# Two matmul pairs of the down products change places: the g_lo products of the main accumulators go behind the g_hi products of the rest accumulators

## The chip, the cores and the metric

The kernel runs on one core of a Trainium2 chip. The core has a matrix engine (TensorE, PE in the profile, with its weight loads shown apart as PEld), VectorE (DVE), ScalarE (ACT), GpSimd (POOL), and SyncE (SP), which here issues the DMAs. Each engine works through its own queue in order, and the queues meet at semaphores. The metric is the device time of one launch in microseconds; less is better.

## What is computed

Three stages over 8192 tokens of width 192. First a causal convolution over 7 tokens with one softmax weight per head and tap, then two feed-forward layers of width 2048 with different activations, in fp32:

```python
out = np.einsum('hk,bskhg->bshg', w, x_unf)          # 7 taps, 8 heads
h = x @ w_in                                         # layer 1: 192 -> 2048
g = np.where(pos, h, np.where(neg, 0.0, (h + beta) ** 2 / (4.0 * beta)))
x = g @ w_out                                        # 2048 -> 192
h = x @ w_in2                                        # layer 2
g = h * (1.0 / (1.0 + np.exp(-1.702 * h)))
return (g @ w_out2).astype(np.float32)
```

## The kernel before

The tokens are cut into 16 tiles of 512. Everything lies transposed: features on the partitions, tokens along the free axis. A feed-forward layer takes 16 steps per tile, one for every 128 of its 2048 hidden features. A step has an up product (into one of the PSUM banks `h`), the activation, and a down product that adds into two banks which last for the whole tile: `main` for output features 0 to 127 and `rest` for the remaining 64.

To keep fp32 precision with the faster fp32r matmuls, operands are split in a rounded part (hi) and a residue (lo). ScalarE rounds the activated tile to g_hi, VectorE subtracts to get g_lo. A down step is then main += w_main g_hi + w_lo g_hi + w_main g_lo, and rest += w_rest g_hi + w_rest g_lo (`w_rest` holds hi and lo weights side by side in 128 columns).

Layer 2 runs `BEHIND` = 24 steps behind layer 1. After the first 24 steps both layers are at work in every slot, and TensorE pairs them. It does not use its 128 rows for one product: the contraction over 128 partitions is cut into LOWER (partitions 0 to 63) and UPPER (64 to 127), and each matmul uses 64 rows. While LOWER works on layer 1, UPPER works on layer 2, and in the second half of a product they change over. In the code the two matmuls of such a pair stand one behind the other (`main1`, `main2`, ...). Since one layer's two halves add into the same bank, the second half of a bank may begin only when the other rows' last matmul on that bank is done. This is what the semaphores `main_half`, `main2_half`, `rest_half` and `rest2_half` are for.

In a slot TensorE does `end_up` (10 matmuls: second half of the up products), `begin_up` (8: first half of the next ones) and `down_both` (20: both halves of the down products, for steps two slots back, `LAG`). `down_both` is lines 616 to 676. The first half of the down products is L634 to L660: L634, L647, L650, L655 and L659 are LOWER (layer 1), L646, L648, L652, L658 and L660 are UPPER (layer 2). The second half is L664 to L676, where layer 1 is UPPER (L664, L667, L669, L672, L675) and layer 2 LOWER (L666, L668, L670, L674, L676). The order within each queue is written out by hand; no scheduler has a part in it.

Who feeds the down step: ScalarE's `round_gate1` (L796) writes g_hi of layer 1, VectorE's `residue1` (L976) writes g_lo of layer 1 and raises `g1_lo_ready`, `residue2` (L982) g_lo of layer 2 and `g2_lo_ready`. At the first step of a tile the bank `main1` must have been read by VectorE (L992) and `rest1` too (L996, y_part), both counted by `y_from_dve`; for layer 2 `out_copied` and `out_summed` do this. GpSimd computes the convolution for the tile after next alongside, in bursts.

`down_both` runs 231 times: 6 slots ahead of the loop, 192 in the loop (6 passes of two tiles with 16 slots each), and 33 behind it.

Of the kernel before, what the change touches and what calls it, by code (L numbers as in the profile page):

```python
# [19 lines left out]
def conv_mlp_mlp(nc, x, conv_w, w_in1, w_out1, w_in2, w_out2, out):  # L20
# [42 lines left out]
    with ExitStack() as ctx:  # L63
# [3 lines left out]
        def sem(name):  # L67
            return ctx.enter_context(nc.semaphore(name))
# [70 lines left out]
        g1_lo_ready = sem("g1_lo_ready")  # L139
# [5 lines left out]
        main_half = sem("main_half")  # L145
        rest_half = sem("rest_half")
        main2_half = sem("main2_half")
# [3 lines left out]
        g2_lo_ready = sem("g2_lo_ready")  # L151
# [60 lines left out]
        LOWER, UPPER = slice(0, DR), slice(DR, P)  # L212
# [94 lines left out]
        def chunk_of(m, kind, c):  # L307
            return m * N_CHUNKS + CHUNKS.index((kind, c))
# [202 lines left out]
        def _(pe):  # L511
# [104 lines left out]
            def down_both(one, two):  # L616

                first1, last1 = one.s == 0, one.s == F_TILES - 1
                first2, last2 = two.s == 0, two.s == F_TILES - 1
                w1, w2 = w_down[0][:, one.s, :], w_down[1][:, two.s, :]  # L620
                hi1, lo1 = g1_hi[one.s % G_RING], g1_lo[one.s % G_RING]
                hi2, lo2 = g2_hi[two.s % G_RING], g2_lo[two.s % G_RING]
                w1_main, w1_rest, w1_lo = w1[:, 0:DM], w1[:, DM:DM + 2 * DR], w1[:, D + DR:2 * D]
                w2_main, w2_rest, w2_lo = w2[:, 0:DM], w2[:, DM:DM + 2 * DR], w2[:, D + DR:2 * D]
                main1, rest1 = (t[:, :] for t in acc1)
                main2, rest2 = (t[:, :] for t in acc2)
                later2 = not isinstance(two.n, int) or two.tile > 0

                pe.wait_ge(g1_hi_ready, one.n + 1)

                pe.wait_ge(down1_done, one.n)
                if first1:
                    pe.wait_ge(y_from_dve, one.tile * 3 - 2)
                nc.tensor.matmul(main1, w1_main[LOWER, :], hi1[LOWER, :], start=first1, stop=False)  # L634
                if isinstance(two.n, int) and two.tile == 0 and two.s % OUT_CHUNK == 0:
                    pe.wait_ge(wp_ready, chunk_of(1, "out", two.s // OUT_CHUNK) + 1 - DVE_CHUNKS)
                pe.wait_ge(g2_hi_ready, two.n + 1)
                if later2 or two.s > 0:

                    pe.wait_ge(down2_done, two.n)  # L640
                else:

                    pe.wait_ge(x_from_dve, 4)
                if first2 and later2:
                    pe.wait_ge(out_copied, two.tile * 2 - 1)
                nc.tensor.matmul(main2, w2_main[UPPER, :], hi2[UPPER, :], start=first2, stop=False)  # L646
                nc.tensor.matmul(main1, w1_lo[LOWER, :], hi1[LOWER, :], start=False, stop=False)  # L647
                nc.tensor.matmul(main2, w2_lo[UPPER, :], hi2[UPPER, :], start=False, stop=False)  # L648
                pe.wait_ge(g1_lo_ready, one.n + 1)
                nc.tensor.matmul(main1, w1_main[LOWER, :], lo1[LOWER, :], start=False, stop=False).then_inc(main_half, 1)  # L650
                pe.wait_ge(g2_lo_ready, two.n + 1)
                nc.tensor.matmul(main2, w2_main[UPPER, :], lo2[UPPER, :], start=False, stop=False).then_inc(main2_half, 1)  # L652
                if first1:
                    pe.wait_ge(y_from_dve, one.tile * 3 - 1)
                nc.tensor.matmul(rest1, w1_rest[LOWER, :], hi1[LOWER, :], start=first1, stop=False)  # L655
                if first2 and later2:
                    pe.wait_ge(out_summed, two.tile)
                nc.tensor.matmul(rest2, w2_rest[UPPER, :], hi2[UPPER, :], start=first2, stop=False)  # L658
                nc.tensor.matmul(rest1, w1_rest[LOWER, :], lo1[LOWER, :], start=False, stop=False).then_inc(rest_half, 1)  # L659
                nc.tensor.matmul(rest2, w2_rest[UPPER, :], lo2[UPPER, :], start=False, stop=False).then_inc(rest2_half, 1)  # L660


                pe.wait_ge(main_half, one.n - (BEHIND - 1))
                nc.tensor.matmul(main1, w1_main[UPPER, :], hi1[UPPER, :], start=False, stop=False)  # L664
                pe.wait_ge(main2_half, two.n + 1)
                nc.tensor.matmul(main2, w2_main[LOWER, :], hi2[LOWER, :], start=False, stop=False)  # L666
                nc.tensor.matmul(main1, w1_lo[UPPER, :], hi1[UPPER, :], start=False, stop=False)  # L667
                nc.tensor.matmul(main2, w2_lo[LOWER, :], hi2[LOWER, :], start=False, stop=False)  # L668
                nc.tensor.matmul(main1, w1_main[UPPER, :], lo1[UPPER, :], start=False, stop=last1)  # L669
                nc.tensor.matmul(main2, w2_main[LOWER, :], lo2[LOWER, :], start=False, stop=last2)  # L670
                pe.wait_ge(rest_half, one.n - (BEHIND - 1))
                nc.tensor.matmul(rest1, w1_rest[UPPER, :], hi1[UPPER, :], start=False, stop=False)  # L672
                pe.wait_ge(rest2_half, two.n + 1)
                nc.tensor.matmul(rest2, w2_rest[LOWER, :], hi2[LOWER, :], start=False, stop=False)  # L674
                nc.tensor.matmul(rest1, w1_rest[UPPER, :], lo1[UPPER, :], start=False, stop=last1).then_inc(down1_done, 1)  # L675
                nc.tensor.matmul(rest2, w2_rest[LOWER, :], lo2[LOWER, :], start=False, stop=last2).then_inc(down2_done, 1)  # L676

# [65 lines left out]
            def slot(tile, side, s):  # L743
                if is_solo(tile, s):
                    solo_slot(tile, side, s)
                    return
                n = tile * F_TILES + s if isinstance(tile, int) else None
                if n is not None and n >= ALL_STEPS:
                    tail_slot(tile, side, s)
                    return  # L750
                if n is None or n > BEHIND:
                    end_up(back(tile, side, s, 1), back(tile, side, s, BEHIND + 1))
                begin_up(back(tile, side, s, 0), back(tile, side, s, BEHIND))
                if n is None or n >= BEHIND + LAG:
                    down_both(back(tile, side, s, LAG), back(tile, side, s, BEHIND + LAG))

            def tail_slot(tile, side, s):
                n = tile * F_TILES + s
                two = back(tile, side, s, BEHIND)
                if n == ALL_STEPS:  # L760
                    end_up(back(tile, side, s, 1), back(tile, side, s, BEHIND + 1))
                    down_both(back(tile, side, s, LAG), back(tile, side, s, BEHIND + LAG))
                if two is not None:
                    up2(two)
                if n == ALL_STEPS + 1:
                    down1(back(tile, side, s, LAG))
                if n > ALL_STEPS:
                    down2(back(tile, side, s, BEHIND + LAG))
# [404 lines left out]
```

## Time and profile before

| | us |
|---|---|
| median of 3 runs | 1221.22 (1221.20 to 1223.06) |
| profiled execution, whole | 1221.22 |
| profiled execution, span | 1219.4 |
| PE busy | 1178.3 (97%) |
| PEld busy | 1067.6 (88%) |
| DVE busy | 889.0 (73%) |
| ACT busy | 819.7 (67%) |
| POOL busy | 471.4 (39%) |

The mean granted TensorE clock was 0.988 of full speed, with the lower values in the first slices. The table's shares are averages over the whole span. A matmul row gives the start and a modelled end; matmuls overlap in the array (each of 0.39 us, one begun every 0.23 us in each half of the rows), so what tells the pace is the distance between starts in one half, not the busy time. A weight load (PEld) has the line of the matmul that it belongs to.

### The profile page before, as it was taken

The numbers are of one execution on the slowest core, as the hardware profiler recorded it, in microseconds if no ns is written. First come the engines' busy times: TensorE is split into PE (matmuls) and PEld (weight loads), VectorE is DVE, ScalarE is ACT, GpSimd is POOL, SyncE is SP. The second block draws the span as 40 slices with busy tenths as digits, with TensorE's granted clock in tenths as the row PEclk, the third lists the DMA queues.
The fourth block names the chain that finished last, engine by engine and source line by source line (L and its number), as shares of the span: only waits on it lengthen the run. The fifth ranks groups of instructions, "written<-read, shape, count | busy, mean of one in ns | idle before, by whom it ended". The sixth has DMA issues, their size and how long they took to land.

```text
span 1219.4 us, 25844 instructions
## 1 busy us (share of the span) xinstructions
PE 1178.3 (97%) x9326; PEld 1067.6 (88%) x9326; DVE 889.0 (73%) x1205; ACT 819.7 (67%) x1545; POOL 471.4 (39%) x426
## 2 busy tenths in 40 slices
PE   7998899999999999999999999999999999999995
PEld 3776798999989899898989989899998989999974
DVE  6976768687786877869687786868778696766532
ACT  5866676776757677685766758576675767765542
POOL 5859818054170714508072360906327080000000
PEclk8999899999999999999999999999999999999998
DMA  7221010101010010101001010000101000000001
GB/s 173 74 67 59 1 34 12 36 1 47 1 46 1 9 39 1 47 1 23 25 7 41 1 47 1 14 33 4 44 1 46 2 11 5 3 13 1 14 10 17
DMA packets 63569, 30.87 MB, mean 25 GB/s; under 512 B 56052, under 2 KB 60274, under 8 KB 63472
## 3 DMA queue, kind: packets, MB, share of 16 engines
q1 hardware_dynamic: 63472, 29.40, 9.5%
q8 instruction: 82, 1.34, 0.4%
q14 instruction: 15, 0.12, 0.0%
HBM read 23.09 MB, written 6.29 MB: 24 GB/s over the span
## 4 chain that ended last, share of the span: by engine, by line
PE 70%; DVE 10%; ACT 7%; issue 6%; POOL 5%; DMA 1%; DVEq 0%; SPq 0%; ACTq 0%; POOLq 0%
ACT clip L790 3%; DVE g_lo L976 3%; DVE g_lo L982 3%; PE acc L650 3%; PE acc L634 2%; PE acc L676 2%; PE acc L655 2%; PE acc L659 2%; PE acc L668 2%; PE acc L674 2%; PE acc L670 2%; PE acc L666 2%; DVE clip L961 2%; PE h L604 2%; PE h L576 2%
## 5 line engine op out<-in xcount | busy, mean ns | idle before, releaser
L790 ACT ACTIVATE clip<-clip,half 128x512 f32<-128x512 f32 x256 | 186.1, 727 | 126.1 <-DVE clip L961 116.8
L970 DVE TENSOR_TENSOR gate<-h,clip 128x512 f32<-128x512 f32 x232 | 160.5, 692 | 143.5 <-ACT clip L790 139.4
L804 ACT ACTIVATE g_hi<-h 128x512 fp32r<-128x512 f32 x256 | 153.5, 600 | 141.9 <-PE h L613 114.5
L982 DVE TENSOR_TENSOR g_lo<-gate,g_hi 128x512 fp32r<-128x512 f32 x256 | 214.9, 839 | 34.0 <-ACT gate L808 34.0
L976 DVE TENSOR_TENSOR g_lo<-gate,g_hi 128x512 fp32r<-128x512 f32 x232 | 223.5, 963 | 18.6 <-ACT g_hi L796 4.4
L961 DVE TENSOR_SCALAR clip<-h 128x512 f32<-128x512 f32 x256 | 175.2, 684 | 84.4 <-PE h L611 79.3
L423 POOL TENSOR_TENSOR x_conv<-x_in,tap_w 128x384 f32<-128x384 f32 (+2 forms) x30 | 26.3, 897 | 499.7 <-ACT raw L844 496.6
L430 POOL TENSOR_TENSOR x_conv<-x_conv,prod 128x384 f32<-128x384 f32 (+2 forms) x180 | 215.9, 1218 | 1.6
L796 ACT ACTIVATE g_hi<-gate 128x512 fp32r<-128x512 f32 x232 | 147.1, 634 | 79.0 <-DVE gate L970 74.4
L423 POOL TENSOR_TENSOR prod<-x_in,tap_w 128x384 f32<-128x384 f32 (+2 forms) x180 | 193.6, 1096 | 8.0 <-DMA x_in<-in_x 3.3
L808 ACT ACTIVATE gate<-h 128x512 f32<-128x512 f32 x256 | 148.7, 581 | 0.0
L844 ACT ACTIVATE raw<-x_conv 32x128 f32<-32x128 f32 x336 | 103.8, 309 | 6.2 <-POOL x_conv L430 1.6
L650 PE MATMUL acc<-g_lo,w_down 64*128 64x512 f32 x231 | 95.8, 415 | 4.4 <-DVE g_lo L976 4.3
L652 PE MATMUL acc<-g_lo,w_down 64*128 64x512 f32 x231 | 95.2, 412 | 0.0
L634 PE MATMUL acc<-g_hi,w_down 64*128 64x512 f32 x231 | 92.2, 399 | 1.7 <-ACT g_hi L796 1.6
L646 PE MATMUL acc<-g_hi,w_down 64*128 64x512 f32 x231 | 91.8, 397 | 0.0
L664 PE MATMUL acc<-g_hi,w_down 64*128 64x512 f32 x231 | 90.8, 393 | 0.0
L659 PE MATMUL acc<-g_lo,w_down 64*128 64x512 f32 x231 | 90.8, 393 | 0.0
L668 PE MATMUL acc<-g_hi,w_down 64*128 64x512 f32 x231 | 90.6, 392 | 0.0
L667 PE MATMUL acc<-g_hi,w_down 64*128 64x512 f32 x231 | 90.6, 392 | 0.0
L655 PE MATMUL acc<-g_hi,w_down 64*128 64x512 f32 x231 | 90.6, 392 | 0.0
L660 PE MATMUL acc<-g_lo,w_down 64*128 64x512 f32 x231 | 90.6, 392 | 0.0
(253 smaller groups left out, 4798.1 us busy)
## 6 DMA issues: line engine op xcount, KB each, us to landing
x_in<-in_x SPq DMA_DIRECT2D x14, 960.0 KB, 4.7
out_y<-raw SPq DMA_DIRECT2D x384, 16.0 KB, 1.4
raw<-in_moe_w_out SPq DMA_DIRECT2D x6, 384.0 KB, 3.3
raw<-in_moe_w_in SPq DMA_DIRECT2D x4, 512.0 KB, 7.5
raw<-in_moe_w_in SPq DMA_DIRECT2D x8, 256.0 KB, 7.2
stage<-in_moe_w_out SPq DMA_DIRECT2D x2, 384.0 KB, 15.1
x_in<-in_x SPq DMA_DIRECT2D x1, 768.0 KB, 4.7
x_in<-in_x SPq DMA_DIRECT2D x2, 283.5 KB
```

What stands on the lines that cost most here:

```text
L423: ins = nc.gpsimd.tensor_tensor(by_head(dst, j), by_head(x_in, at + j), w, ALU.mult)
L430: ins = nc.gpsimd.tensor_tensor(o, o, prod[k % 2][:, j:j + slabs, 0:width], ALU.add)
L634: nc.tensor.matmul(main1, w1_main[LOWER, :], hi1[LOWER, :], start=first1, stop=False)
L650: nc.tensor.matmul(main1, w1_main[LOWER, :], lo1[LOWER, :], start=False, stop=False).then_inc(main_half, 1)
L790: nc.scalar.activation(c, c, ACT.Square, bias=half[:, :], scale=0.5).then_inc(square_ready, 1)
L796: nc.scalar.activation(g1_hi[step.s % G_RING][:, :], gate1_of(step)[:, :], ACT.Copy).then_inc(g1_hi_ready, 1)
L804: nc.scalar.activation(g2_hi[step.s % G_RING][:, :], src, ACT.Gelu_apprx_sigmoid).then_inc(g2_hi_ready, 1)
L808: nc.scalar.activation(gate2[:, :], src, ACT.Gelu_apprx_sigmoid).then_inc(gate2_ready, 1)
L961: nc.vector.tensor_scalar(clip[step.s % 2][:, :], bank1(step)[:, :], -1.0, 1.0, ALU.max, ALU.min).then_inc(clip_ready, 1)
L970: nc.vector.tensor_tensor(gate1_of(step)[:, :], bank1(step)[:, :], clip[step.s % 2][:, :], ALU.max).then_inc(gate1_ready, 1)
L976: nc.vector.tensor_tensor(g1_lo[k][:, :], gate1_of(step)[:, :], g1_hi[k][:, :].bitcast(FP32), ALU.subtract).then_inc(g1_lo_ready, 1)
L982: nc.vector.tensor_tensor(g2_lo[k][:, :], gate2[:, :], g2_hi[k][:, :].bitcast(FP32), ALU.subtract).then_inc(g2_lo_ready, 1)
```

## The change

In `down_both`, in the first half, the pair of g_lo products into the main banks (with the waits for `g1_lo_ready` and `g2_lo_ready`, and with the increments of `main_half` and `main2_half`) moves behind the pair of g_hi products into the rest banks (with their waits at a tile's first step). In the second half the same pairs change places, there without waits of their own on g_lo; the waits for `rest_half` and `rest2_half` move ahead with the rest pair. No instruction is added or removed.

```diff
--- before.py
+++ after.py
@@ -646,16 +646,16 @@
                 nc.tensor.matmul(main2, w2_main[UPPER, :], hi2[UPPER, :], start=first2, stop=False)
                 nc.tensor.matmul(main1, w1_lo[LOWER, :], hi1[LOWER, :], start=False, stop=False)
                 nc.tensor.matmul(main2, w2_lo[UPPER, :], hi2[UPPER, :], start=False, stop=False)
-                pe.wait_ge(g1_lo_ready, one.n + 1)
-                nc.tensor.matmul(main1, w1_main[LOWER, :], lo1[LOWER, :], start=False, stop=False).then_inc(main_half, 1)
-                pe.wait_ge(g2_lo_ready, two.n + 1)
-                nc.tensor.matmul(main2, w2_main[UPPER, :], lo2[UPPER, :], start=False, stop=False).then_inc(main2_half, 1)
                 if first1:
                     pe.wait_ge(y_from_dve, one.tile * 3 - 1)
                 nc.tensor.matmul(rest1, w1_rest[LOWER, :], hi1[LOWER, :], start=first1, stop=False)
                 if first2 and later2:
                     pe.wait_ge(out_summed, two.tile)
                 nc.tensor.matmul(rest2, w2_rest[UPPER, :], hi2[UPPER, :], start=first2, stop=False)
+                pe.wait_ge(g1_lo_ready, one.n + 1)
+                nc.tensor.matmul(main1, w1_main[LOWER, :], lo1[LOWER, :], start=False, stop=False).then_inc(main_half, 1)
+                pe.wait_ge(g2_lo_ready, two.n + 1)
+                nc.tensor.matmul(main2, w2_main[UPPER, :], lo2[UPPER, :], start=False, stop=False).then_inc(main2_half, 1)
                 nc.tensor.matmul(rest1, w1_rest[LOWER, :], lo1[LOWER, :], start=False, stop=False).then_inc(rest_half, 1)
                 nc.tensor.matmul(rest2, w2_rest[UPPER, :], lo2[UPPER, :], start=False, stop=False).then_inc(rest2_half, 1)
 
@@ -666,12 +666,12 @@
                 nc.tensor.matmul(main2, w2_main[LOWER, :], hi2[LOWER, :], start=False, stop=False)
                 nc.tensor.matmul(main1, w1_lo[UPPER, :], hi1[UPPER, :], start=False, stop=False)
                 nc.tensor.matmul(main2, w2_lo[LOWER, :], hi2[LOWER, :], start=False, stop=False)
-                nc.tensor.matmul(main1, w1_main[UPPER, :], lo1[UPPER, :], start=False, stop=last1)
-                nc.tensor.matmul(main2, w2_main[LOWER, :], lo2[LOWER, :], start=False, stop=last2)
                 pe.wait_ge(rest_half, one.n - (BEHIND - 1))
                 nc.tensor.matmul(rest1, w1_rest[UPPER, :], hi1[UPPER, :], start=False, stop=False)
                 pe.wait_ge(rest2_half, two.n + 1)
                 nc.tensor.matmul(rest2, w2_rest[LOWER, :], hi2[LOWER, :], start=False, stop=False)
+                nc.tensor.matmul(main1, w1_main[UPPER, :], lo1[UPPER, :], start=False, stop=last1)
+                nc.tensor.matmul(main2, w2_main[LOWER, :], lo2[LOWER, :], start=False, stop=last2)
                 nc.tensor.matmul(rest1, w1_rest[UPPER, :], lo1[UPPER, :], start=False, stop=last1).then_inc(down1_done, 1)
                 nc.tensor.matmul(rest2, w2_rest[LOWER, :], lo2[LOWER, :], start=False, stop=last2).then_inc(down2_done, 1)
```

First place, TensorE's queue in the first half of `down_both` in a loop slot, from the third pair on. acc1_0 is main1, acc1_1 rest1, acc2_0 main2, acc2_1 rest2. Before:

```order
L650 MATMUL acc1_0<-g1_lo1,w_down1 128x512 [waits g1_lo_ready]
L652 MATMUL acc2_0<-g2_lo1,w_down2 128x512 [waits g2_lo_ready]
L655 MATMUL acc1_1<-g1_hi1,w_down1 128x512
L658 MATMUL acc2_1<-g2_hi1,w_down2 128x512
L659 MATMUL acc1_1<-g1_lo1,w_down1 128x512
L660 MATMUL acc2_1<-g2_lo1,w_down2 128x512
```

and now (the lines are those of the changed file):

```order
L651 MATMUL acc1_1<-g1_hi1,w_down1 128x512
L654 MATMUL acc2_1<-g2_hi1,w_down2 128x512
L656 MATMUL acc1_0<-g1_lo1,w_down1 128x512 [waits g1_lo_ready]
L658 MATMUL acc2_0<-g2_lo1,w_down2 128x512 [waits g2_lo_ready]
L659 MATMUL acc1_1<-g1_lo1,w_down1 128x512
L660 MATMUL acc2_1<-g2_lo1,w_down2 128x512
```

The pair that waits for g_lo stood third and stands fourth; the next pair to wait, for `main_half` and `main2_half`, stood three pairs behind it and now stands two pairs behind it.

Second place, the same queue right behind, the second half of `down_both`. Before:

```order
L664 MATMUL acc1_0<-g1_hi1,w_down1 128x512 [waits main_half]
L666 MATMUL acc2_0<-g2_hi1,w_down2 128x512 [waits main2_half]
L667 MATMUL acc1_0<-g1_hi1,w_down1 128x512
L668 MATMUL acc2_0<-g2_hi1,w_down2 128x512
L669 MATMUL acc1_0<-g1_lo1,w_down1 128x512
L670 MATMUL acc2_0<-g2_lo1,w_down2 128x512
L672 MATMUL acc1_1<-g1_hi1,w_down1 128x512 [waits rest_half]
L674 MATMUL acc2_1<-g2_hi1,w_down2 128x512 [waits rest2_half]
L675 MATMUL acc1_1<-g1_lo1,w_down1 128x512
L676 MATMUL acc2_1<-g2_lo1,w_down2 128x512
```

and now:

```order
L664 MATMUL acc1_0<-g1_hi1,w_down1 128x512 [waits main_half]
L666 MATMUL acc2_0<-g2_hi1,w_down2 128x512 [waits main2_half]
L667 MATMUL acc1_0<-g1_hi1,w_down1 128x512
L668 MATMUL acc2_0<-g2_hi1,w_down2 128x512
L670 MATMUL acc1_1<-g1_hi1,w_down1 128x512 [waits rest_half]
L672 MATMUL acc2_1<-g2_hi1,w_down2 128x512 [waits rest2_half]
L673 MATMUL acc1_0<-g1_lo1,w_down1 128x512
L674 MATMUL acc2_0<-g2_lo1,w_down2 128x512
L675 MATMUL acc1_1<-g1_lo1,w_down1 128x512
L676 MATMUL acc2_1<-g2_lo1,w_down2 128x512
```

The rest pair with its two waits stood fourth of five and stands third; the last pair, whose end frees the operands and the banks, is where it was.

## Rows read from the trace of the kernel before

**Rows 1.** The page: busy us, share of the span, instructions of each engine.
```profile
PE 1178.3 (97%) x9326; PEld 1067.6 (88%) x9326; DVE 889.0 (73%) x1205; ACT 819.7 (67%) x1545; POOL 471.4 (39%) x426
```

**Rows 2.** The page, costliest groups: the g_lo matmul of LOWER.
```profile
L650 PE MATMUL acc<-g_lo,w_down 64*128 64x512 f32 x231 | 95.8, 415 | 4.4 <-DVE g_lo L976 4.3
```

**Rows 3.** Timeline of a quiet slot: start us, duration us, engine, line, operation.
```profile
600.86 0.39 PE L634 MATMUL acc<-g_hi,w_down 64*128 64x512 f32 x1
...
601.10 0.39 PE L647 MATMUL acc<-g_hi,w_down 64*128 64x512 f32 x1
...
601.41 0.39 PE L652 MATMUL acc<-g_lo,w_down 64*128 64x512 f32 x1
...
601.79 0.39 PE L659 MATMUL acc<-g_lo,w_down 64*128 64x512 f32 x1
601.86 0.18 PEld L666 LDWEIGHTS acc<-g_hi,w_down 64*128 64x128 f32 x1
601.88 0.39 PE L660 MATMUL acc<-g_lo,w_down 64*128 64x512 f32 x1
...
602.03 0.39 PE L666 MATMUL acc<-g_hi,w_down 64*128 64x512 f32 x1
...
602.11 0.39 PE L664 MATMUL acc<-g_hi,w_down 64*128 64x512 f32 x1
...
605.30 0.39 PE L634 MATMUL acc<-g_hi,w_down 64*128 64x512 f32 x1
```

**Rows 4.** List of waits, of weight loads: us in total, times, longest.
```profile
PEld acc L650 <- DVE g_lo L976: 21.9, 64, 0.9
```

**Rows 5.** Timeline of the slot with the longest wait of a tile.
```profile
560.18 0.39 PE L647 MATMUL acc<-g_hi,w_down 64*128 64x512 f32 x1
...
560.88 0.18 PEld L650 LDWEIGHTS acc<-g_lo,w_down 64*128 64x128 f32 x1 [0.74 <-DVE g_lo L976]
560.88 0.50 PE L650 MATMUL acc<-g_lo,w_down 64*128 64x512 f32 x1 [0.31 <-DVE g_lo L976]
560.89 0.18 PEld L652 LDWEIGHTS acc<-g_lo,w_down 64*128 64x128 f32 x1
...
561.23 0.39 PE L655 MATMUL acc<-g_hi,w_down 64*128 64x512 f32 x1
```

**Rows 6.** Timeline of the slot after it.
```profile
565.19 0.39 PE L647 MATMUL acc<-g_hi,w_down 64*128 64x512 f32 x1
...
565.38 0.18 PEld L650 LDWEIGHTS acc<-g_lo,w_down 64*128 64x128 f32 x1 [0.23 <-DVE g_lo L976]
...
565.72 0.39 PE L655 MATMUL acc<-g_hi,w_down 64*128 64x512 f32 x1
```

**Rows 7.** Timeline of PE: start and end of the waiting slots.
```profile
555.42 0.39 PE L634 MATMUL acc<-g_hi,w_down 64*128 64x512 f32 x1
...
578.21 0.39 PE L590 MATMUL h<-x_rest_a,rest_hi 64*128 64x512 f32 x1
```

**Rows 8.** Timeline of VectorE, its g_lo of the first layer.
```profile
539.98 0.69 DVE L976 TENSOR_TENSOR g_lo<-gate,g_hi 128x512 fp32r<-128x512 f32 x1
...
545.12 0.69 DVE L976 TENSOR_TENSOR g_lo<-gate,g_hi 128x512 fp32r<-128x512 f32 x1
...
559.33 1.50 DVE L976 TENSOR_TENSOR g_lo<-gate,g_hi 128x512 fp32r<-128x512 f32 x1
...
563.83 1.50 DVE L976 TENSOR_TENSOR g_lo<-gate,g_hi 128x512 fp32r<-128x512 f32 x1
...
572.82 1.50 DVE L976 TENSOR_TENSOR g_lo<-gate,g_hi 128x512 fp32r<-128x512 f32 x1
```

**Rows 9.** Timeline of the slot that begins a token tile in rest1.
```profile
578.47 0.67 DVE L996 TENSOR_TENSOR y_part<-acc,y_part 64x512 f32<-64x512 f32 x1
...
578.94 0.39 PE L647 MATMUL acc<-g_hi,w_down 64*128 64x512 f32 x1
...
579.19 0.18 PEld L655 LDWEIGHTS acc<-g_hi,w_down 64*128 64x128 f32 x1
```

## The prediction

> **What bounds the kernel now.** I read the page first for the engine that fills the span. TensorE is busy 1178.3 us of 1219.4 [rows 1], VectorE 73%, so any time lost or won on TensorE's queue counts at once, while the others have room. Next I read the timeline of one quiet slot (one pass of the PE queue: end of an up product, start of the next, and the 20 down matmuls) [rows 3]. From one L634 to the next are 605.30 - 600.86 = 4.44 us. That is 38 matmuls, 19 in each half of the array (LOWER rows 0 to 63, UPPER rows 64 to 127), and the halves run side by side: 4.44 / 19 = 0.234 us from one matmul to the next in the same half. The reader should see in these rows that L634 (600.86) and L647 (601.10) are both LOWER and 0.24 apart, that the UPPER half follows 0.08 us later (L659 at 601.79, L660 at 601.88), and that nothing idles. So a quiet slot is at its floor, and only two things can move the time: a stall that goes and a stall that comes.
>
> The stalls that are there I took from the list of waits: the weight load of L650 waits for VectorE's g_lo in 64 slots, 21.9 us in all [rows 4]. It is one of 231 such slots [rows 2]. The wait stands at the weight load, not at the matmul; that matters below. I then looked at the worst such slot [rows 5] and a mild one [rows 6] to learn what a late load costs:
> - Worst: L647 starts at 560.18, the load of L650 only at 560.88, and L655, two places on, at 561.23 instead of 560.18 + 0.47 = 560.65. So a load is followed by the next matmul of its half but one 0.35 us later; with the usual 0.234 taken off, a matmul really streams about 0.115 us after its load begins.
> - Mild: load 0.19 late (565.38 after 565.19), L655 at 565.72, which is 0.53 after L647 instead of 0.47: 0.06 lost. The same rule gives 0.19 + 0.115 - 0.234 = 0.07.
> The rule I take: a load may start up to 0.12 us after the matmul before it in its half at no cost; every ns beyond that is lost.
> A second thing in rows 5: L652 is UPPER and waits for another semaphore, yet its load starts at 560.89, 0.01 after L650's. Waits are taken in program order, and one held load holds those behind it in both halves.
>
> How much these stalls are worth in a tile of 16 slots: from L634 at 555.42 to L590 at 578.21 [rows 7] lie five slots less one matmul, 94 intervals of 0.234 = 21.9 to 22.0 us; they took 22.79. About 0.8 us per tile is lost, over 64 / 5 = 13 tiles (five waiting slots each): 10.4 us, the most that moving L650 can give back.
>
> **What the change removes.** The g_lo matmul moves behind the hi matmul of the rest accumulator, in each half one interval later, so it tolerates 0.23 us more lateness of VectorE. The lower bound of the gain is this one shift per tile, since the lateness of a tile is one run of slots: 13 x 0.23 = 3.0 us. The upper bound is all of it, 10.4 us. Which one depends on who sets the pace in these slots. VectorE does [rows 8]: its g_lo (L976) takes 0.69 us early and 1.50 us later. It ends at 540.67 (539.98 + 0.69) and, four slots on, at 560.83 (559.33 + 1.50): 5.04 us per slot, 0.6 more than TensorE's 4.44, so VectorE falls behind. After that it runs at (572.82 - 563.83) / 2 = 4.50. If TensorE's own slot grows to 4.54 (next part), 4 x 0.1 = 0.4 us less lateness comes together in the four slots, and VectorE's 4.50 is then the faster of the two. With the 0.23 of the shift that is 0.63, against the 0.58 lost in the worst slot (1.05 - 0.47) [rows 5]. So I take all of it: -10.4 us.
>
> **What the change adds.** The second half of the down products may touch an accumulator's bank only when the first half's last matmul on it is done: L664 (UPPER) waits for main_half, L666 (LOWER) for main2_half. In the quiet slot [rows 3] L652 starts at 601.41, ends at 601.80, and the load of L666 starts at 601.86: 0.45 after L652, and 0.07 after L659, its neighbour in LOWER. It is waiting already, inside the free 0.12. After the change L650 and L652 start one interval (0.234) later and L664, L666 stay where they are. Step by step, with T the start of L634 in its half: the g_lo matmul starts at T + 3 x 0.234 = T + 0.70; the load that waits for it at T + 1.15; the matmul streams from T + 1.265; its place was T + 5 x 0.234 = T + 1.17. Lost: 0.10 us. With the present lead of 0.08 of LOWER over UPPER the first such slot costs LOWER 0.17 and UPPER 0.02, which brings the halves level or over; since a held load holds both, they settle level, at 0.10 each in every slot. Bounds per slot: 0 (if a late load cost nothing) and 0.17 (if the lagging half set the pace every time). I take 0.10, by the nearest rows, those of 5 and 6: 231 x 0.10 = +23.1 us.
>
> The Trainium skill, page "TensorE: Matmul & The Clock Gate", section "Architectural detail: the array is 16× 32×32, not 1× 128×128", says that a matmul can begin before its weight load has finished. By that alone the late load would be free. The record agrees as to the start (L650 is recorded at 560.88 with its load [rows 5]) but it lasts 0.50 instead of 0.39 and the next matmul comes 0.35 after the load, so the measurement decides for a cost.
>
> The waits of the rest accumulators: rest_half comes at the same matmul as before (L659), its waiter moves one interval ahead. L659 at T + 0.93, plus 0.45 = T + 1.38; the load's place is T + 1.40 without, T + 1.50 with the new stall. It costs 0 while the stall before it covers it.
>
> Once a tile, rest1's first matmul waits for y_part (L996) and is now one interval earlier. L996 ends at 578.47 + 0.67 = 579.14 [rows 9], and L655's load starts at 579.19. In the new place it would be due at L647's start, 578.94: 0.25 late, less the free 0.12 = 0.13; 13 to 14 tiles, x 0.12 = +1.6 us. Bounds 0 and 14 x 0.23 = 3.2. The wait of rest2 for out_summed is due earlier by as much, and no such wait is in the list, so 0. Loads, matmuls, DMAs and the work of the other engines stay the same in number. The last pair of the second half keeps its place, so down1_done and down2_done, on which ScalarE waits, do not move within a slot.
>
> Sum: +23.1 - 10.4 + 1.6 = +14.3 us. The profiled execution took 1221.22 (1219.4 span and 1.8 around it), the same as the median, so 1221.2 + 14.3 = 1235.5. In the first few down slots TensorE waits for others anyway, which may hide up to 7 x 0.10 = 0.7.
>
> **The rivals.**
> - A, faster: the late load of the second half costs nothing. For it: the load would be 0.21 late, still inside the 0.234 interval. It decides if the load may be hidden up to 0.23 instead of 0.12. Then +23.1 and the y_part cost go, VectorE keeps its pace of 4.50 in five slots, and only the shift is won: 1221.2 - 3.0 = 1218.2. Against it: rows 6, where 0.19 late cost 0.06. The sentence of the Trainium skill cited above would lead here. Chance 0.06.
> - B, much slower: the halves do not settle level; the one that lags pays 0.17 in every slot and the other waits for it. 231 x 0.17 = 39.3, - 10.4 + 1.6 = +30.5: 1251.7. Against it: the halves have separate streams in rows 3. Chance 0.06.
> - C, about the same: the completion signal is nearer than 0.45 because the last matmul on a bank drains while others run, and the stall is 0.04: 231 x 0.04 = 9.2, - 8 + 1 = +2: 1223.4. Here TensorE stays faster than 4.50, so less than 10.4 is won back. Chance 0.06.
> - D: the stall is as forecast but VectorE still is late and only 3.0 is won: 1221.2 + 23.1 - 3.0 + 1.6 = 1242.9. For it: the 0.63 of slack against 0.6 needed is thin. Chance 0.12, with all between it and the forecast.
>
> **How the numbers follow.** Forecast 0.70, its own range 1230 to 1240 (0.08 to 0.12 per slot). The range reaches to D: 1228 to 1243; A, B and most of C are left out. 0.2% is 2.4 us, about what a measurement of this kernel can tell from no change. Faster: A, 0.05. Same: the weak end of A and half of C, 0.04. Slower: the rest, 0.91.
>
> **What would show it.** A quiet slot, L634 to L634, at 4.53 to 4.54 us instead of 4.44. The loads of L664 and L666 0.21 after the matmul before them in their half (0.45 after the moved g_lo matmuls), the halves nearly level. The list of waits with little or nothing for g_lo at the moved matmul, and new waits at L664 and L666 for matmuls of TensorE itself. VectorE's total busy time as before. The forecast is wrong if a quiet slot still takes 4.44 us (then A), or over 4.6 (then B); if it takes 4.53 and g_lo is still waited for, it is D.

## The result, and the profile after

| | before | changed |
|---|---|---|
| median, us | 1221.68 (4 runs) | 1236.43 (4 runs) |
| ratio | | 1.0116, 95% interval 1.0099 to 1.0134 |
| span of the profiled execution | 1219.4 | 1235.4 |

The change costs 14.8 us. 1235.5 was forecast, with a range of 1228 to 1243.

The page of the changed kernel: first the busy times (answers to [rows 1]), then the costliest groups (line, engine, operation, tiles, count | busy us, mean ns | idle before, releaser).

```profile
PE 1198.1 (97%) x9326; PEld 1040.4 (84%) x9326; DVE 890.0 (72%) x1205; ACT 817.4 (66%) x1545; POOL 471.3 (38%) x426
...
L666 PE MATMUL acc<-g_hi,w_down 64*128 64x512 f32 x231 | 115.3, 499 | 0.0
L664 PE MATMUL acc<-g_hi,w_down 64*128 64x512 f32 x231 | 113.7, 492 | 0.0
...
L664 PEld LDWEIGHTS acc<-g_hi,w_down 64*128 64x128 f32 x231 | 42.4, 184 | 59.7 <-PE acc L656 59.6
```

TensorE's matmuls are "busy" 20 us longer, but not because there is more to do: the count is the same. L666 and L664 have a mean of 499 and 492 ns where a matmul that nothing holds has 391, because the record of a matmul whose load came late begins with the load. The third of these group rows tells why the loads come late: 59.7 us of idle weight-load time before L664, ended by L656, which is a matmul of TensorE itself.

The list of waits of the weight loads (us in total, times, longest), against [rows 4]:

```profile
PEld acc L664 <- PE acc L656: 59.6, 230, 0.3
...
PEld acc L651 <- DVE y_part L996: 2.5, 11, 0.2
...
PEld acc L656 <- DVE g_lo L976: 1.8, 5, 0.6
...
PEld acc L634 <- DVE y_lo_a L992: 1.2, 6, 0.2
...
PEld acc L634 <- DVE y_lo_b L992: 1.0, 5, 0.2
```

The wait for g_lo was 21.9 us in 64 slots and is 1.8 in 5 (it stands at L656 now). In its place is a wait of TensorE for its own other half, 59.6 us in 230 of 231 slots. Before, a tile's first slot waited at L634 for y_lo longer than now, and not at all for y_part:

```profile
PEld acc L634 <- DVE y_lo_b L992: 2.7, 6, 0.5
PEld acc L634 <- DVE y_lo_a L992: 2.6, 6, 0.4
```

How late g_lo comes is seen best in the slot with the longest wait of a tile. First the kernel before, where the g_lo of rows 8 ends at 559.33 + 1.50 = 560.83, then the same slot of the changed kernel:

```profile
559.95 0.39 PE L634 MATMUL acc<-g_hi,w_down 64*128 64x512 f32 x1
```

```profile
565.95 1.50 DVE L976 TENSOR_TENSOR g_lo<-gate,g_hi 128x512 fp32r<-128x512 f32 x1
567.07 0.39 PE L634 MATMUL acc<-g_hi,w_down 64*128 64x512 f32 x1
```

Before, g_lo is ready 0.88 us after the slot's L634; now 565.95 + 1.50 - 567.07 = 0.38 after it. That is 0.50 less, and the load that needs it is due 0.47 after L634 now instead of 0.23.

A quiet slot of the changed kernel (start us, duration us, engine, line, operation), against [rows 3]:

```profile
621.81 0.39 PE L646 MATMUL acc<-g_hi,w_down 64*128 64x512 f32 x1
...
621.85 0.39 PE L634 MATMUL acc<-g_hi,w_down 64*128 64x512 f32 x1
...
622.55 0.39 PE L656 MATMUL acc<-g_lo,w_down 64*128 64x512 f32 x1
...
622.75 0.39 PE L660 MATMUL acc<-g_lo,w_down 64*128 64x512 f32 x1
...
623.00 0.18 PEld L664 LDWEIGHTS acc<-g_hi,w_down 64*128 64x128 f32 x1 [0.26 <-PE acc L656]
623.00 0.49 PE L664 MATMUL acc<-g_hi,w_down 64*128 64x512 f32 x1
623.03 0.18 PEld L666 LDWEIGHTS acc<-g_hi,w_down 64*128 64x128 f32 x1
623.03 0.50 PE L666 MATMUL acc<-g_hi,w_down 64*128 64x512 f32 x1
...
623.34 0.39 PE L667 MATMUL acc<-g_hi,w_down 64*128 64x512 f32 x1
...
623.37 0.39 PE L668 MATMUL acc<-g_hi,w_down 64*128 64x512 f32 x1
...
626.40 0.39 PE L634 MATMUL acc<-g_hi,w_down 64*128 64x512 f32 x1
```

The g_lo matmul on main of layer 1's first half, L656, starts at 622.55, and the load that waits for it at 623.00: 0.45 later, as the held load in [rows 3]. The load stands 0.25 after the matmul before it in its half (L660, 622.75), and the next matmul of the half, L667, comes 0.34 after the load. From L660 to L667 are 0.59 instead of 0.47: 0.12 lost. UPPER is 0.03 to 0.04 us ahead of LOWER through the slot, and the two held loads start 0.03 apart. From L634 (621.85) to L634 (626.40) are 4.55 us.

**All slots.** Over the 230 intervals between the 231 slots, from the rows of L634 (min/median/max duration, then first and last start us), before and changed:

```profile
L634 PE MATMUL acc<-g_hi,w_down x231: 390/391/625, 97.2 to 1143.0; 64*128 64x512 f32 x116
```

```profile
L634 PE MATMUL acc<-g_hi,w_down x231: 390/392/789, 98.1 to 1159.0; 64*128 64x512 f32 x116
```

1143.0 - 97.2 = 1045.8 us before, 1159.0 - 98.1 = 1060.9 now: 15.1 of the 16.0 us of span lie here. The mean slot is 4.547 and 4.613; the median of the same intervals, which leaves out the stalls of once a tile, is 4.434 and 4.553.

### The profile page after: what moved, and what is told of

The parts are those of the page before. It is cut to its first block, busy times and chain, and to the rows that moved or that the text cites. A ratio compares the mean times of both kernels' runs of the same rounds, so it can differ in the third digit from the quotient of the medians.

```text
span 1235.4 us, 25844 instructions
## 1 busy us (share of the span) xinstructions
PE 1198.1 (97%) x9326; PEld 1040.4 (84%) x9326; DVE 890.0 (72%) x1205; ACT 817.4 (66%) x1545; POOL 471.3 (38%) x426
## 4 chain that ended last, share of the span: by engine, by line
PE 89%; POOL 5%; ACT 2%; DVE 2%; DMA 1%; issue 1%; SPq 0%; POOLq 0%; ACTq 0%; DVEq 0%
PE acc L664 6%; PE acc L673 4%; PE h L587 4%; PE h L607 4%; PE acc L675 4%; PE h L605 4%; PE h L589 4%; PE h L609 4%; PE h L585 4%; PE acc L670 4%; PE h L611 4%; PE h L602 4%; PE h L592 4%; PE acc L648 4%; PE acc L667 3%; PE acc L646 3%
## 5 line engine op out<-in xcount | busy, mean ns | idle before, releaser
L976 DVE TENSOR_TENSOR g_lo<-gate,g_hi 128x512 fp32r<-128x512 f32 x232 | 223.7, 964 | 19.3 <-ACT g_hi L796 5.2
L666 PE MATMUL acc<-g_hi,w_down 64*128 64x512 f32 x231 | 115.3, 499 | 0.0
L664 PE MATMUL acc<-g_hi,w_down 64*128 64x512 f32 x231 | 113.7, 492 | 0.0
L634 PE MATMUL acc<-g_hi,w_down 64*128 64x512 f32 x231 | 91.5, 396 | 2.5 <-ACT g_hi L796 2.5
L664 PEld LDWEIGHTS acc<-g_hi,w_down 64*128 64x128 f32 x231 | 42.4, 184 | 59.7 <-PE acc L656 59.6
L651 PE MATMUL acc<-g_hi,w_down 64*128 64x512 f32 x231 | 92.4, 400 | 0.0
L646 PE MATMUL acc<-g_hi,w_down 64*128 64x512 f32 x231 | 91.8, 398 | 0.0
L658 PE MATMUL acc<-g_lo,w_down 64*128 64x512 f32 x231 | 91.5, 396 | 0.0
L656 PE MATMUL acc<-g_lo,w_down 64*128 64x512 f32 x231 | 91.0, 394 | 0.3 <-DVE g_lo L976 0.2
L654 PE MATMUL acc<-g_hi,w_down 64*128 64x512 f32 x231 | 91.2, 395 | 0.0
L648 PE MATMUL acc<-g_hi,w_down 64*128 64x512 f32 x231 | 91.2, 395 | 0.0
```

Source lines behind the costliest of these rows:

```text
L976: nc.vector.tensor_tensor(g1_lo[k][:, :], gate1_of(step)[:, :], g1_hi[k][:, :].bitcast(FP32), ALU.subtract).then_inc(g1_lo_ready, 1)
```

## The experiments

The first four ran on one chip together. "One wait instead of two" (both_waits below), "The new order in the waiting slots alone" (late_slots_only) and "VectorE's lateness taken away at its source" (x_early) shared a second chip, "The pair swapped" and "The change and the earlier x together" a third. A ratio compares with the kernel before on the same chip. The diffs are shortened: `...` stands for what is left out, and so do comments; waits that go along with a matmul are not all printed.

### First half alone

```diff
-                nc.tensor.matmul(main1, ..., lo1[LOWER, :], ...).then_inc(main_half, 1)
-                nc.tensor.matmul(main2, ..., lo2[UPPER, :], ...).then_inc(main2_half, 1)
                 nc.tensor.matmul(rest1, ..., hi1[LOWER, :], ...)
                 nc.tensor.matmul(rest2, ..., hi2[UPPER, :], ...)
+                nc.tensor.matmul(main1, ..., lo1[LOWER, :], ...).then_inc(main_half, 1)
+                nc.tensor.matmul(main2, ..., lo2[UPPER, :], ...).then_inc(main2_half, 1)
```

> Only the first half of the down products is reordered (g_lo pair of main behind the g_hi pair of rest), the second half as before. Theory (the bank handover at L664 and L666 is what costs): all of the cost is here, a quiet slot of 4.55 us as in the changed kernel, g_lo no longer waited for, about 1236 us (1234 to 1238). Rival (the alternation between banks in each half costs some 0.06 us per half): 4.49 us per slot and about 1229.

Measured: 1235.5 us, ratio 1.0118 (1.0101 to 1.0134). The waits of its weight loads:

```profile
PEld acc L664 <- PE acc L656: 59.3, 230, 0.3
```

All of the cost is in the first half's order: the wait is the changed kernel's (59.6), and the median slot is 4.547 us. The rival falls.

### Second half alone

```diff
-                nc.tensor.matmul(main1, ..., lo1[UPPER, :], ..., stop=last1)
-                nc.tensor.matmul(main2, ..., lo2[LOWER, :], ..., stop=last2)
                 nc.tensor.matmul(rest1, ..., hi1[UPPER, :], ...)
                 nc.tensor.matmul(rest2, ..., hi2[LOWER, :], ...)
+                nc.tensor.matmul(main1, ..., lo1[UPPER, :], ..., stop=last1)
+                nc.tensor.matmul(main2, ..., lo2[LOWER, :], ..., stop=last2)
```

> Only the second half is reordered, the first as before. Theory: rest_half and rest2_half are signalled 0.45 us after L659 and L660, at T+1.38 and T+1.46, and the loads that wait are due at T+1.40, inside the free 0.12 us: nothing lost, slot 4.43, g_lo waited for as before (about 22 us in 64 slots), 1221 to 1223 us. Rival (alternation costs in each half): about 1229.

Measured: 1221.6 us, ratio 1.0001 (0.9992 to 1.0011). The wait for g_lo is as it was:

```profile
PEld acc L650 <- DVE g_lo L976: 22.2, 65, 0.8
```

The second half's order and the rest accumulators' earlier waits cost nothing: the median slot stays 4.434 us.

### One place further

```diff
 # first half, against the kernel before; the g_hi pair of rest now follows directly here
-                pe.wait_ge(g1_lo_ready, one.n + 1)
-                nc.tensor.matmul(main1, ..., lo1[LOWER, :], ...).then_inc(main_half, 1)
-                pe.wait_ge(g2_lo_ready, two.n + 1)
-                nc.tensor.matmul(main2, ..., lo2[UPPER, :], ...).then_inc(main2_half, 1)
 ...
+                pe.wait_ge(g1_lo_ready, one.n + 1)
                 nc.tensor.matmul(rest1, ..., lo1[LOWER, :], ...).then_inc(rest_half, 1)
+                pe.wait_ge(g2_lo_ready, two.n + 1)
                 nc.tensor.matmul(rest2, ..., lo2[UPPER, :], ...).then_inc(rest2_half, 1)
+                nc.tensor.matmul(main1, ..., lo1[LOWER, :], ...).then_inc(main_half, 1)
+                nc.tensor.matmul(main2, ..., lo2[UPPER, :], ...).then_inc(main2_half, 1)
```

> First half: the g_lo pair of main goes one more place back, behind the g_lo pair of rest, so that the bank is handed over with one pair between instead of two; second half as before. Theory (signal 0.45 us after the last matmul on the bank, then 0.12 us free): one interval of 0.234 us more per slot than in the changed kernel, 4.79 us per slot, 1236 + 54 = 1290 us (1285 to 1295). Rival (a fixed cost of any wait that is met late, whatever the distance): 1236.

Counted from the pair that signals to the pair that waits, the distance is three pairs in the kernel before, two in the changed kernel and one here. So two pairs, one and none stand between them; the expectation above, and the one of the next experiment, count one too many where they say "between".

Measured: 1283.19 us (one run). In a quiet slot (L659 is the last matmul on main of LOWER here):

```profile
618.55 0.39 PE L634 MATMUL acc<-g_hi,w_down 64*128 64x512 f32 x1
...
619.49 0.39 PE L659 MATMUL acc<-g_lo,w_down 64*128 64x512 f32 x1
619.93 0.18 PEld L664 LDWEIGHTS acc<-g_hi,w_down 64*128 64x128 f32 x1 [0.48 <-PE acc L659]
...
623.33 0.39 PE L634 MATMUL acc<-g_hi,w_down 64*128 64x512 f32 x1
```

The load of L664 starts 0.44 after L659, and the slot takes 4.78 us: 0.23 more than the changed kernel's (4.55). By the medians it is 4.773 against 4.553. Taking one pair out of the distance costs about one interval, and the signal keeps its way of 0.44 to 0.45. The time came 7 us lower than forecast: 231 x 0.22 is 51 instead of 54, and the rest fits the once-a-tile stalls that are left in the changed kernel: the wait for y_part, 2.5 us in 11 slots there, is 0.2 in one here.

### Distance restored

```diff
 # down_both, between its two halves, on top of the change; end_up later leaves this pair out
+                pe.wait_ge(h1_half, one.n - (BEHIND - 1))
+                nc.tensor.matmul(bank_1, in_hi[0][UPPER, cols1], x_hi[UPPER, :], start=False, stop=False)
+                pe.wait_ge(h2_half, two.n + 1)
+                nc.tensor.matmul(bank_2, in_hi[1][LOWER, cols2], y_hi[LOWER, :], start=False, stop=False)
```

> The changed kernel, with the first pair of the next up product's second half (L602, L604) moved between the two halves of the down products, so that main is handed over with three pairs between, as before. Nothing added or removed. Theory: the stall at L664 goes, quiet slot 4.43; g_lo keeps its 0.23 us of tolerance (-3.0), the last down pair ends 0.23 us later, which the handover of a tile's banks to VectorE waits for (+3.0, once a tile), y_part +1.5: 1220 to 1225 us. Rival (the order of the products as such costs): 4.55 per slot and 1236 or more.

Measured: 1224.64 us, ratio 1.003 (1.002 to 1.0039). In a quiet slot (L659 is the g_lo matmul into main of LOWER, L669 the first UPPER matmul of the second half):

```profile
623.88 0.39 PE L659 MATMUL acc<-g_lo,w_down 64*128 64x512 f32 x1
...
624.37 0.18 PEld L669 LDWEIGHTS acc<-g_hi,w_down 64*128 64x128 f32 x1
...
624.60 0.39 PE L669 MATMUL acc<-g_hi,w_down 64*128 64x512 f32 x1
```

L669's load is 0.49 after L659 and the matmul follows 0.23 after its load: not late. The median slot is 4.441 us. 11 of the 15 us are gone although the down products stand in the changed order, so the distance is what costs. The time is at the upper end of what was expected. The wait for g_lo did not shrink:

```profile
PEld acc L659 <- DVE g_lo L983: 22.2, 66, 0.7
```

against 21.9 in 64 before, so the 3.0 us that the forecast gave to the shift did not come. The last down pair ends one interval later here, ScalarE's copy of the output comes after it, and VectorE waits for that copy (L1005; L1012 in this file): 17.8 us in 15 times against 14.5 in 15 before, 0.22 more each time. In the slot with the longest wait g_lo ends 1.10 us after the slot's first down matmul (L983 at 559.37 + 1.50, L637 at 559.77) instead of 0.88. VectorE is later by what the shift gives, and the two cancel. A tile's first load waits longer for y_lo too, 7.3 us in all instead of 5.3.

### One wait instead of two

```diff
                 pe.wait_ge(main_half, one.n - (BEHIND - 1))
-                nc.tensor.matmul(main1, w1_main[UPPER, :], hi1[UPPER, :], start=False, stop=False)
                 pe.wait_ge(main2_half, two.n + 1)
+                nc.tensor.matmul(main1, w1_main[UPPER, :], hi1[UPPER, :], start=False, stop=False)
```

> The changed kernel, but the waits for main_half and main2_half both stand ahead of L664, and L666 has none of its own. The changed kernel's slot is 4.553 us, 0.12 over 4.434, where 0.10 was forecast; its halves stand 0.035 us apart with UPPER ahead, and the held loads of L664 and L666 start 0.034 apart. Theory 1 (two held loads one behind the other are let go 0.034 apart, and the half that is let go last is the one that L664 waits for in the next slot): with one held load the halves come level and the slot shrinks by 0.02 to 0.035, to 4.52 to 4.535, 1229 to 1233 us. Theory 2 (the signal is simply later than 0.45 us): slot 4.55 and 1236 as in the changed kernel.

Measured: 1257.18 us, ratio 1.0293 (1.0271 to 1.0315), 21 us slower than the changed kernel; both theories miss it.

```profile
622.78 0.39 PE L658 MATMUL acc<-g_lo,w_down 64*128 64x512 f32 x1
...
622.82 0.39 PE L656 MATMUL acc<-g_lo,w_down 64*128 64x512 f32 x1
...
623.36 0.18 PEld L665 LDWEIGHTS acc<-g_hi,w_down 64*128 64x128 f32 x1 [0.35 <-PE acc L656]
...
623.39 0.18 PEld L666 LDWEIGHTS acc<-g_hi,w_down 64*128 64x128 f32 x1
...
623.70 0.39 PE L667 MATMUL acc<-g_hi,w_down 64*128 64x512 f32 x1
```

The held load starts 0.54 after L656 instead of 0.45, so two waits ahead of one load cost 0.09 to 0.10 us per slot, x 231 = 21 to 23; the median slot is 4.653. The second signal is not what comes late: L658, which gives it, starts 0.04 before L656. The halves still stand 0.04 apart and the loads 0.03, though only one of them has waits: theory 1 falls. Theory 2 left the number of waits out of account, so this run does not test it.

### The pair swapped

```diff
-                pe.wait_ge(main_half, one.n - (BEHIND - 1))
-                nc.tensor.matmul(main1, w1_main[UPPER, :], hi1[UPPER, :], start=False, stop=False)
                 pe.wait_ge(main2_half, two.n + 1)
                 nc.tensor.matmul(main2, w2_main[LOWER, :], hi2[LOWER, :], start=False, stop=False)
+                pe.wait_ge(main_half, one.n - (BEHIND - 1))
+                nc.tensor.matmul(main1, w1_main[UPPER, :], hi1[UPPER, :], start=False, stop=False)
```

> The changed kernel with L666 (LOWER, layer 2) ahead of L664 (UPPER, layer 1) in the queue, each with its own wait. Theory (of two held loads the second starts 0.034 later whatever it waits for, and in the next slot the first one waits for the half that lags): mirror image, LOWER now 0.035 ahead, slot again 4.55, 1236 us. Rival (the 0.02 over the forecast belongs to UPPER or to main_half's signal): slot 4.53, about 1231.

Measured: 1236.83 us (one run). L664 is the LOWER and L666 the UPPER matmul here, L656 LOWER, L658 UPPER:

```profile
621.85 0.39 PE L656 MATMUL acc<-g_lo,w_down 64*128 64x512 f32 x1
...
621.86 0.39 PE L658 MATMUL acc<-g_lo,w_down 64*128 64x512 f32 x1
...
622.33 0.18 PEld L664 LDWEIGHTS acc<-g_hi,w_down 64*128 64x128 f32 x1 [0.29 <-PE acc L658]
...
622.34 0.18 PEld L666 LDWEIGHTS acc<-g_hi,w_down 64*128 64x128 f32 x1
```

The time is the one forecast, but the picture is not the mirror image: the halves stand level (0.01), and the loads start 0.47 and 0.49 after the matmuls that they wait for. The median slot is the changed kernel's, 4.553. The same 0.03 us is paid, once as a distance between the halves and once as a later signal. What it is stays open.

### The new order in the waiting slots alone

```diff
+                late = one.s in (11, 12, 13, 14, 15)
+                if late:   # with the waits of this pair at a tile's first step
+                    nc.tensor.matmul(rest1, ..., hi1[LOWER, :], ...)
+                    nc.tensor.matmul(rest2, ..., hi2[UPPER, :], ...)
                 nc.tensor.matmul(main1, ..., lo1[LOWER, :], ...).then_inc(main_half, 1)
                 nc.tensor.matmul(main2, ..., lo2[UPPER, :], ...).then_inc(main2_half, 1)
-                nc.tensor.matmul(rest1, ..., hi1[LOWER, :], ...)
-                nc.tensor.matmul(rest2, ..., hi2[UPPER, :], ...)
+                if not late:
+                    nc.tensor.matmul(rest1, ..., hi1[LOWER, :], ...)
+                    nc.tensor.matmul(rest2, ..., hi2[UPPER, :], ...)
```

> Before, with the first half's new order only in the five slots of a tile in which VectorE's g_lo is waited for (layer 1 steps 11 to 15, TensorE slots 13, 14, 15, 0 and 1). Theory: in the worst slot 0.23 of the 0.51 us of stall goes, the five slots pay the 0.12 of the bank handover, but there TensorE stands waiting for VectorE anyway; quiet slots stay at 4.43. Net -0.3 to +0.1 us per tile, 1217 to 1223 us. Rival (the cost of the new order comes on top everywhere): five times 0.12 more per tile, 13 tiles, less 3.0: 1226 or more.

Measured: 1222.76 us, ratio 1.0016 (1.0006 to 1.0027). In its file L660 is the g_lo matmul and L675 the first of the second half:

```profile
PEld acc L675 <- PE acc L660: 18.0, 73, 0.3
PEld acc L660 <- DVE g_lo L987: 8.3, 19, 0.8
```

The wait for g_lo fell from 21.9 to 8.3 us, and 18.0 us of waits for the bank came in 73 slots. The time lies inside the range of the theory, at its upper end, and the median slot is 4.437 us. The new order takes away much of the wait that it was put there for and gives the time back next to it; nothing is won even where it works.

### VectorE's lateness taken away at its source

```diff
-        EARLY = dict(move=..., turn={7: 0, 10: 1}, hi={10: 0, 11: 1},
-                     lo={11: 0, 12: 1})
+        EARLY = dict(move=..., turn={7: 0, 10: 1}, hi={8: 0, 11: 1},
+                     lo={9: 0, 12: 1})
```

> The kernel before, TensorE's order untouched; of the preparation of the next tile's x the rounding of the main part on ScalarE moves from slot 10 to 8 and its residue on VectorE (L1028, 0.75 us) from slot 11 to 9, ahead of the stretch in which GpSimd works and VectorE's g_lo takes 1.5 us. Theory (the wait at L650 is accumulated lateness of VectorE, 0.6 us by slot 14): the lateness shrinks by the 0.7 us that leave the stretch, the wait in slots 13 and 14 goes and most of that in 15 to 1 with it: 0.5 to 0.8 us per tile, 1211 to 1215 us. Rival (VectorE's lateness is set in slot 9 by its wait for the output copy, L1005, and an operation more there makes it worse): 1221 or more.

Measured: 1215.26 us, ratio 0.9958 (0.9945 to 0.9971), faster than both kernels. VectorE (against [rows 8]) and the wait at L650:

```profile
539.18 0.67 DVE L1028 TENSOR_TENSOR x_lo_a<-raw,x_hi_a 128x512 fp32r<-128x512 f32 x1
...
541.50 0.69 DVE L976 TENSOR_TENSOR g_lo<-gate,g_hi 128x512 fp32r<-128x512 f32 x1
...
555.25 1.50 DVE L976 TENSOR_TENSOR g_lo<-gate,g_hi 128x512 fp32r<-128x512 f32 x1
```

```profile
PEld acc L650 <- DVE g_lo L976: 15.0, 54, 0.8
```

L1028 stands in slot 9 now. From the end of the L976 at 541.50 (542.19) to the end of the one at 555.25 (556.75) are three slots of 4.85 us. In the kernel before, the three that end at 560.83 begin at 545.81 [rows 8] and average 5.01. VectorE takes 0.46 us less for three slots. In the worst slot its g_lo ends 0.53 us after L634 (556.75 and 556.22) instead of 0.88, the slot ahead of that one no longer waits, and the wait fell from 21.9 to 15.0 us. The time is 0.3 us above the range that was expected (1211 to 1215); the slots after the worst wait as before, since VectorE runs at 4.50 there.

### The change and the earlier x together

```diff
 # on top of the change
-                     turn={7: 0, 10: 1}, hi={10: 0, 11: 1}, lo={11: 0, 12: 1}
+                     turn={7: 0, 10: 1}, hi={8: 0, 11: 1}, lo={9: 0, 12: 1}
```

> The changed kernel with x_early's edit. Theory (in the changed kernel VectorE is late nowhere any more, all of that gain is taken, and the slot of 4.55 is TensorE's own bank handover): no change against the changed kernel, 1235 to 1237 us, slot 4.553. Rival (part of the changed kernel's time is still VectorE's lateness): as much faster as x_early was, 1230 to 1232.

Measured: 1234.05 us, ratio 1.0106 (1.0088 to 1.0124).

```profile
PEld acc L664 <- PE acc L656: 59.4, 230, 0.3
```

The wait for the bank is the same as in the changed kernel (59.6), and the median slot is 4.547. x_early wins 5.2 us on the old order; here the two medians, taken on different chips, are 2.4 us apart and their ratios' intervals overlap. The list of waits shows what is left to win in the changed kernel: its waits for y_part at L651 (2.5 us) and for y_lo at L634 (2.2 us) are missing here, and the wait for g_lo is 1.8 us in 5 in both. So VectorE's late g_lo costs nothing more in the changed kernel, as the theory had it; its late y_lo and y_part, once a tile, do, by about 2 us. There the theory was wrong.

## Why the prediction was right

- *A load held by a wait may be 0.12 us late at no cost, and what is beyond is lost.* Right. In the changed kernel 0.25 late cost 0.12, where the arithmetic of rows 5 and 6 gives 0.25 + 0.115 - 0.234 = 0.13. It holds further out too: in both_waits the load is 0.35 late (623.36 after L660 at 623.01) and the slot is longer by 0.22, and in "One place further" it is 0.47 late (619.93 after L660 at 619.46) and the slot is longer by 0.34. The sentence of the Trainium skill that a matmul can begin before its load has finished (page "TensorE: Matmul & The Clock Gate", section "Architectural detail: the array is 16× 32×32, not 1× 128×128") agrees with the record of starts and does not carry over to the pace: L664 starts with its load, and L667 comes 0.34 after it. Rival A, which needed it, falls.
- *The bank handover at L664 and L666 is the cost, +23.1 us.* The mechanism is shown: the first half alone has all of it, a distance shorter by one pair costs about one interval more, and one pair put back takes it away. Its size was 0.12 per slot instead of 0.10: 4.553 - 4.434 = 0.119 (medians of the slot, from the starts of L634), x 231 = +27.5. That is the upper end of the forecast's own 0.08 to 0.12, and a quiet slot is 4.55 where 4.53 to 4.54 was named. The forecast was that the halves settle level, with a load 0.45 after its matmul. The halves stand 0.03 apart instead, and where they do stand level, with the pair swapped, the load comes 0.03 later and the slot is the same. Where these 0.03 come from stays open.
- *The stall for VectorE's g_lo goes in full, -10.4 us.* Right: 1.8 us of wait in 5 slots is left of 21.9 in 64. D, which had it stay, falls. The reason is right too. The forecast had TensorE's slower slot take 4 x 0.1 = 0.4 us off VectorE's lateness; 4 x 0.12 = 0.48 would be the same step with the slot as measured, and g_lo comes 0.50 us less late into the worst slot (0.38 after L634, not 0.88). With the 0.23 of the shift that is more than the 0.58 that was lost there. Where the quiet slots stay fast, in late_slots_only, 8.3 us of wait are left in 19 slots.
- *y_part, +1.6 us.* The new wait at L651 is there, 2.5 us in 11 slots, and costs what was forecast. In a tile's first slot of the changed kernel:

```profile
585.04 0.40 PE L590 MATMUL h<-x_rest_a,rest_hi 64*128 64x512 f32 x1
...
585.54 0.38 PE L647 MATMUL acc<-g_hi,w_down 64*128 64x512 f32 x1
...
585.79 0.18 PEld L651 LDWEIGHTS acc<-g_hi,w_down 64*128 64x128 f32 x1 [0.22 <-DVE y_part L996]
...
586.13 0.39 PE L656 MATMUL acc<-g_lo,w_down 64*128 64x512 f32 x1
```

  The load is 0.25 late, and from L647 to L656 are 0.59 instead of 0.47: 0.12 lost.
- *What the sum left out: the wait for y_lo.* Just ahead of that place the load of L634 waits for VectorE's y_lo. In the kernel before:

```profile
578.61 0.18 PEld L634 LDWEIGHTS acc<-g_hi,w_down 64*128 64x128 f32 x1 [0.43 <-DVE y_lo_b L992]
```

  From L590 (578.21) [rows 7] to L647 (578.94) [rows 9] are 0.73 us instead of 0.47: 0.26 lost once a tile. The 0.8 us per tile of the forecast end at L590, just before this stall. In the changed kernel L590 to L647 are 0.50: 0.03 lost, because VectorE comes less late here too. In 13 tiles that is 3.0 us won which no term held.
- *The rest accumulators' waits cost nothing.* Right, by the second half alone: 1.0001. The first half alone costs as much as the whole change, so they cost nothing on top of the new stall either.
- *The sum.* The 230 intervals grew by 15.1 us. 27.5 less 15.1 leaves 12.4 us of stalls gone, where the forecast had 10.4 - 1.6 = 8.8; the y_lo stall of 3.0 is most of the difference. The bank term was too small by 4.4 us and the stalls' by 3.6, and their errors go against each other. The hit to 1 us (14.3 forecast, 14.8 measured) is partly luck, that to 5 us is not.
- Rival B needed halves that do not share the stall; they do. Rival C needed a signal nearer than 0.45 us; it is 0.44 to 0.49 in each of the rows above where a load is held by one wait.

## What to carry to other kernels

When a wait for another engine is moved to a later place in a saturated queue, look at what else the moved instruction signals: here it also hands a bank to the other half of the array, and the one pair that is left between is less than the signal's way. Count the distance from the signalling matmul to the load that waits for it in intervals, set it against the delay that one row of the trace shows (0.45 us), and do it for the quiet slots: a stall of 0.12 us in 231 of them outweighs 0.8 us in each of 13 tiles. If the late engine is late in a known stretch, move work out of that stretch on that engine instead, as x_early does.

## What was not expected of the hardware

- Two semaphore waits ahead of one weight load hold it 0.09 us longer than one: 0.54 us after the matmul waited for, instead of 0.45 (1257.18 against 1236.43 us). What takes this time is not shown.
- At this place of the queue the two held loads of different halves start 0.03 us apart, the halves too, even where the second load has no wait of its own (both_waits). With the order swapped they start 0.01 apart and the first comes 0.02 to 0.03 later after its matmul. The slot is the same, 4.55 us.
